# GpSimd splits the first eight weight tiles, and TensorE makes three unread products ahead of ten level groups

## The reference

```python
def _attn_ref(q, k, v, alpha):            # 4 x 8 heads, 768 tokens, 48 wide
    for t in range(S):
        state = alpha[:, :, t, :, None] * state + einsum('bhd,bhe->bhde', k[:, :, t], v[:, :, t])
        y[:, :, t] = einsum('bhd,bhde->bhe', q[:, :, t], state)

def _moe_ref(x, domain_probs, w1, w2):    # 3072 tokens x 384, 4 experts of 1024
    p = domain_probs / (domain_probs.sum(-1, keepdims=True) + 1e-09)
    for e in range(E):
        out += p[:, e:e + 1] * (maximum(x @ w1[e], 0.0) @ w2[e])

def _moe2_ref(x, w_in, w_out):            # 384 -> 2048 -> 384
    h = x @ w_in
    return (h - tanh(h)) @ w_out
```

## Time and profile before

| | us |
|---|---|
| median of 3 runs | 1374.95 (1374.37 to 1376.28) |
| the profiled execution | 1376.28 |
| its span | 1373.8 |
| TensorE busy | 1346.9 (98%) |
| TensorE on the chain that ended last | 90% |
| VectorE, ScalarE, GpSimd busy | 859.2, 569.1, 280.2 |
| mean granted clock | 0.987 |

### The profile page before, as it was taken

How to read it: one execution, slowest core, us unless ns; L and a number is a source line. 1 busy time by engine, 2 the same in 40 slices (tenths; PEclk the granted TensorE clock), 3 DMA queues, 4 the chain that set the end, 5 groups by cost and what they waited for, 6 DMA issues and landing times.

```text
span 1373.8 us, 26614 instructions
## 1 busy us (share of the span) xinstructions
PE 1346.9 (98%) x10589; PEld 1130.7 (82%) x10589; DVE 859.2 (63%) x1698; ACT 569.1 (41%) x1063; POOL 280.2 (20%) x270
## 2 busy tenths in 40 slices
PE   5899999999999999999999999999999999999999
PEld 5778788988878888878898888898887889888888
DVE  6874856985644975464787464497555478333385
ACT  1426256833233841414662323474231476111185
POOL 4767653014031002313001304000221000000000
PEclk7799999999999999999999999999999999999999
DMA  7497896866565656656655655655665465655552
GB/s 228 109 357 252 286 326 234 312 223 219 192 209 196 227 182 215 202 187 208 236 192 178 216 189 196 227 212 184 215 203 164 163 225 195 213 189 202 181 192 87
DMA packets 104682, 289.22 MB, mean 211 GB/s; under 512 B 9936, under 2 KB 64304, under 8 KB 104560
## 3 DMA queue, kind: packets, MB, share of 16 engines
q1 hardware_dynamic: 104128, 287.22, 62.3%
q10 hardware_dynamic: 432, 0.31, 0.1%
HBM read 242.61 MB, written 42.52 MB: 208 GB/s over the span
## 4 chain that ended last, share of the span: by engine, by line
PE 90%; DVE 6%; issue 2%; POOL 1%; DMA 1%; ACT 0%; DVEq 0%; SPq 0%; POOLq 0%; ACTq 0%
PE bank L742 15%; PE bank L743 13%; PE bank L744 13%; PE bank L767 9%; PE bank L768 9%; PE bank L769 9%; PE bank L793 4%; PE bank L791 4%; PE bank L792 4%; PE bank L633 3%; PE bank L691 1%; DVE RG L1265 1%; PE bank L611 1%; PE bank L663 1%; PE bank L653 1%
## 5 line engine op out<-in xcount | busy, mean ns | idle before, releaser
L967 ACT ACTIVATE HH<-GG 128x512 fp32r<-128x512 f32 x192 | 121.2, 631 | 630.5 <-PE bank L769 509.3
L742 PE MATMUL bank<-XB,RG 128*128 128x512 f32 x864 | 349.1, 404 | 3.5 <-DMA XB<-XS 3.1
L743 PE MATMUL bank<-XB,RG 128*128 128x512 f32 x864 | 340.0, 393 | 0.0
L744 PE MATMUL bank<-XB,RG 128*128 128x512 f32 x864 | 339.0, 392 | 0.0
L1215 DVE SCALAR_TENSOR_TENSOR GG<-bank,PB 128x512 f32<-128x512 f32 x192 | 133.4, 695 | 312.3 <-PE bank L744 312.0
L767 PE MATMUL bank<-HH,RG 128*128 128x512 f32 x576 | 224.3, 389 | 0.0
L768 PE MATMUL bank<-HH,RG 128*128 128x512 f32 x576 | 224.2, 389 | 0.0
L769 PE MATMUL bank<-HL,RG 128*128 128x512 f32 x576 | 224.0, 389 | 0.0
L1420 POOL TENSOR_TENSOR KU<-KU,TOT 128x256 f32<-128x256 f32 x80 | 62.2, 805 | 686.3 <-PE bank L633 686.3
L742 PEld LDWEIGHTS bank<-XB,RG 128*128 128x128 f32 x864 | 162.4, 188 | 44.4 <-issue 3.3
L744 PEld LDWEIGHTS bank<-XB,RG 128*128 128x128 f32 x864 | 162.5, 188 | 35.5
(11 more groups left out here) (121 smaller groups left out, 1687.6 us busy)
## 6 DMA issues: line engine op xcount, KB each, us to landing
RG<-scratch SPq DMA_DIRECT2D x240, 768.0 KB, 4.3
scratch<-RG SPq DMA_DIRECT2D x48, 768.0 KB, 5.3
VS<-vp SPq DMA_DIRECT2D x11, 768.0 KB, 6.1
WS<-w SPq DMA_DIRECT2D x32, 192.0 KB, 3.6
PB<-probs SPq DMA_DIRECT2D x6, 1024.0 KB, 6.9
AU<-qka SPq DMA_DIRECT2D x11, 512.0 KB, 5.4
R<-qka SPq DMA_DIRECT2D x11, 512.0 KB, 5.6
KU<-qka SPq DMA_DIRECT2D x11, 512.0 KB, 6.3
```

The lines of the kernel that those rows point to most:

```text
L742: nc.tensor.matmul(out, w1(g, 0, kt), x_part(m, 0, kt), start=(kt == order[0]), stop=False)
L743: nc.tensor.matmul(out, w1(g, 0, kt), x_part(m, 1, kt), start=False, stop=False)
L744: last = nc.tensor.matmul(out, w1(g, 1, kt), x_part(m, 0, kt), start=False, stop=(kt == order[-1]))
L967: nc.scalar.activation(HH[:, h_slot(g)], GG[:, h_slot(g)], ACT.Copy).then_inc(high, 1)
```

## The change

1. `paired_scores` takes its two bank waits first, and for levels 1 to 5 of both units it then makes three products of the identity with itself (128x128, float32, `keep_clock`) into the bank that the group's second half overwrites, ahead of the waits for keys and queries. Ten groups, thirty products.
2. The second run of unread products, ahead of the layers, grows from 6 to 12.
3. VectorE's splits 2 and 3 go to GpSimd, which now does 0 to 7 itself.
4. GpSimd multiplies unit 2's queries (`spread_queries(AHEAD)`) ahead of `join(1)`, not in `prepare(2)`. `join(1)` waits for that in place of the two waits on `keys_up`. `prepare(2)` no longer waits for unit 1's carried states between the two spreads.

```diff
             def paired_scores(u, level):
+                bank_free(u, 2 + 2 * level)
+                bank_free(u, 3 + 2 * level)
                 if level == 0:
                     pe.wait_ge(spread[own(u)], 1)
                 else:
+                    keep_clock(fill_bank(u, 3 + 2 * level), 3)
                     pe.wait_ge(keys_up[own(u)], level)
                     pe.wait_ge(rotated[own(u)], level)
-                bank_free(u, 2 + 2 * level)
-                bank_free(u, 3 + 2 * level)
...
-            keep_clock(bank[4], 6)
+            keep_clock(bank[4], 12)
...
             states(1)
-            split_low(2)
-            split_low(3)
             low_x(0)
...
-                spread_queries(u)
-                if pause:
-                    pool.wait_ge(carried[own(u - 1)], pause)
+                if u > AHEAD:
+                    spread_queries(u)
                 spread_distant(u)
...
             def join(u):
-                pool.wait_ge(keys_up[0], NL)
-                pool.wait_ge(keys_up[1], NL)
+                pool.wait_ge(spread[0], 2)
...
+            spread_queries(AHEAD)
             join(1)
             pool.wait_ge(joined[1], 5)
             split_low(0)
             split_low(1)
-            prepare(2, carried_at(1))
-            for g in range(LEAD, RING):
+            prepare(AHEAD)
+            for g in range(2, RING):
                 split_low(g)
```

More of the change, by code:

```diff
@@ L637, in scores, with keep_clock @@
                             last.then_inc(filled[own(u)], 1)
+            def keep_clock(out, n):
+                for i in range(n):
+                    nc.tensor.matmul(out[:, 0:P], ident[:, :], ident[:, :], start=True, stop=True)
             def paired_scores(u, level):
+                bank_free(u, 2 + 2 * level)
+                bank_free(u, 3 + 2 * level)
                 if level == 0:
@@ L694, in attend @@
                 last.then_inc(filled[own(u)], 1)
-            def keep_clock(out, n):
-                for i in range(n):
-                    nc.tensor.matmul(out[:, 0:P], ident[:, :], ident[:, :], start=True, stop=True)
             def attention(u, step):
@@ L1261, in split_low @@
             def split_low(g):
-                if g in (2, SLOTS1 + LEAD):
+                if g == SLOTS1 + LEAD:
                     dve.wait_ge(w_low, g)
@@ L1398, in paired_tabulate, with prepare @@
                     nc.gpsimd.tensor_tensor(both, one, two, ALU.mult).then_inc(tabled[own(u)], 1)
-            def prepare(u, pause=0):
+            def prepare(u):
                 n = turn_of(u)
@@ L1451, in split_low @@
             def split_low(g):
-                if g == LEAD:
-                    pool.wait_ge(w_low, g)
                 pool.wait_ge(w_high, g + 1)
```

## The result

The changed kernel takes 1385.93 us (median of four runs, 1385.66 to 1387.23) against 1374.92 (1374.37 to 1376.28) for the kernel before on the same chip: 11.0 us slower by the medians; the ratio is given as 1.0074, interval 1.0062 to 1.0086, which is 8.5 to 11.8 us. The forecast was 1375.3. What happened is the rival called "the clock stays at half until the transposes", and it cost more than the 8.2 us that it was priced at. The profiled execution of before is the slowest of its four, so the two profiles lie only 9.9 apart in their spans.

The account below looks back on a forecast made before the run. TensorE, busy 98% of the span, bounds the kernel after the start. GpSimd raising unit 2's keys at 79.5 against 79.14 adds 0.35 us to the 1374.95 median: 1375.3, own range 1373.8 to 1376.9, 8-in-10 range 1372.2 to 1383.4.

Parts of the forecast that it names:

- the clock stays at half until the transposes: Slower rival, TensorE's score groups: products run at half clock, last score 9 or more later; +8.2 us, 1383.2; chance 0.20.
- Step 3: TensorE's clock in the score groups: three wide products between narrow groups bring full clock back by the early thirties.
- The rival's price: Half-clock case: ten groups' products cost 12.8 to 15 us, pauses hide 3.9; last score 9 later, level 1 +8.2.
- Step 1: TensorE up to 28.5 us: nothing moves in time, two pauses (3.4 us) hide the first four groups' products.
- Step 2: TensorE from 28.48 to the last score: instruction supply of 126 rows per 3.9 us; end at 42.2, 0.7 later.
- Step 4: VectorE gives away its two splits; first wide products at full clock, TensorE alone about 2.4 us sooner after five tiles.
- the 3.97: Time in us of VectorE's two weight splits, said to go from the chain of waits before the first wide product.
- Step 5: GpSimd, the deciding part: join 1.1 late, more work behind it, unit 2's keys raised at 79.5, TensorE then takes level 1.
- +0.75 and +0.5: GpSimd behind the join: queries gone (minus 3.10), two splits of 1.92 added, +0.75; late staging of weight tiles, +0.5.
- the sum: Whole change at level 1 of unit 2: 79.5 against 79.14, +0.35 us, give or take 1.5.

Follow-up runs that it names:

- e2: Kernel before with only the thirty unread products and the bank waits ahead of them; 1386.38 us, ratio 1.0069.
- e3: Changed kernel with six unread products ahead of each of the ten groups instead of three; 1381.76 us (one run), kernel before 1376.14.
- e8: Changed kernel with fourteen unread products ahead of the first group, three ahead of the nine others; 1380.15 us (one run), kernel before 1376.51.
- e12: Kernel before with unit 2's queries ahead of the join, fourteen products ahead of the first group, three ahead of each other; 1375.96 us, ratio 1.0001.
- e4: Changed kernel with fourteen unread products ahead of the first group, none ahead of the others; 1381.45 us (one run), kernel before 1376.14.
- e9: Kernel before with unit 2's queries ahead of the join, fourteen products ahead of the first group, one ahead of each other; 1378.89 us, ratio 1.0015.
- e1: Changed kernel without the thirty unread products ahead of the groups; 1376.89 us, ratio 1.0007.
- e5: Changed kernel without the thirty products, with unit 2's queries and the join's waits back in their old places; 1380.69 us, ratio 1.0030.
- e6: Kernel before with one edit, GpSimd multiplies unit 2's queries ahead of the join; 1374.72 us, ratio 0.9991.
- e11: The kernel of e6 run again, unchanged, in a later comparison; 1374.04 us, ratio 0.9986.
- e10: Kernel of e6 with one more wait: GpSimd starts unit 2's queries only after unit 1's last keys are raised; 1376.73 us, ratio 1.0002.

## Why the prediction was wrong, step by step

**Step 3, the clock: the step that failed.** "Now three wide products stand between any two narrow groups, as in neither of the two, so I take the clock to be back by the early thirties." It was at half to the end of the transposes near 56. The argument took a place between two known ends (scores alone, 128-column work alone) and put it at the upper one without a row. What the runs showed in its place: three per group left it at half for 34 us, in the traces of after and e2 (and each of their eight executions took 1384.97 or more), six per group brought it up (e3). Once it was full, three kept it (e8, e12); it fell under groups alone in e4 and with one per group in e9. So the clock that this pattern ran at depended on the clock that it found. Products are not all of it: in e1 and e5 plain groups reached the full clock. The rival that the clock stays at half had 0.20 and was the better reading of the one row that counted, twelve microseconds of narrow work at half.

**The rival's price.** It was right in kind and too low: 9 for 10.8 at the last score, 8.2 for 9.7 at level 1 of unit 2, 8.2 for 11.0 on the median. Its own terms, 12.8 to 15 less 3.9, gave 8.9 to 11.1 for the last score; it took the lowest. Six product rows at half take 1.58 (17.86 to 19.43 on the chain), above the 1.28 to 1.5 taken from eight transposes and a 512-column product; ten are 15.8. Of these 5.0 were hidden (15.8 - 10.8), the pauses and short waits, about the 3.9 set down for them, and at the join nothing more was.

**Step 1** said that nothing moves up to 28.5 since the pauses hide four groups' products "about" at half. In after group (1,2) starts at 29.68, so its row 27, which stood at 28.48, comes near 30.5: 2 us late. The pauses themselves did vanish, as said. Its price for three products at full clock was too low as well: 2.06 for 16 rows is 0.77 for six, not 0.73, and e8 has 0.86 (23.80 to 24.66).

**Step 2** took 3.9 us per 126 product rows as the limit of the instruction supply. In e12 TensorE ran 505 product rows from 29.14 to 43.91, 3.7 us per 126, with one pause of 0.27 in them, and its own pace was 1.93 per 70 rows, 3.5 per 126. The limit is no higher than 3.7 there; it would have made the forecast 0.6 smaller and was no part of the miss. Two slips in the step have no weight either: group (0,5) ends 70 rows before the last, not 76, and 104 rows of the mix at its own prices take 2.3, not 2.0. By the Trainium skill, "Runtime: NRT & Kernel Launch", "Instruction fetch mechanics", the crossing of a block is mostly hidden. Inside the score groups and away from the loading of the first 30 us these runs agree, with pauses of 0.2 to 0.3; during it the runs with few or no products between the groups don't, with 0.9 to 3.2. That these pauses are such crossings rests on the count of 126 rows alone.

**Step 4.** VectorE's two splits left, and the first wide product came at full clock as said. What was wrong is the 3.97: on their own they are 1.99, the rest was GpSimd's doing, and moving the queries alone gives that back (e6, e11).

**Step 5.** The mechanism held: GpSimd worked without a pause from the join to the keys, and TensorE waited 1.98 for them (2 to 3 forecast). The sum was +0.75 and +0.5 behind the join: 88.76 - 55.47 is 33.3, against 32.7 before, so +0.6 and not +1.25: six splits cost 4.2 more than four and the queries' 3.1 are gone, but the first distant query took 1.6 where it had taken 2.13, and no staging wait came through. The join itself was to be +1.1 from step 2 alone; e1 shows +1.9 with no delay of the scores at all. It was the contention that the step left out: it let the queries run "into this idle time" of GpSimd without asking who shares something with GpSimd in it. e1, the change without its products, came out 0.75 above its kernel before where the sum had +0.35; that is the forecast about right by luck, two errors that cancel: TensorE's scores were not late, and the rotation was. The interval of e1 takes in no difference, so it can't confirm the sum either.

**The measure.** The kernel before spreads from 1374.2 to 1379.2 over all comparisons, and part of that has a source that the traces show: the two pauses ahead of 23 and 29 us were 1.38 and 2.06 in one run, 0.92 and 1.78 in e6, 1.20 and 3.15 in e10, with nothing changed ahead of them. The groups behind them start up to a microsecond earlier or later. Places of different profiles are therefore compared by their distances (join behind last score), not by their times alone.

## What to carry to other kernels

Beyond the 5 us of pauses that they filled, the unread products were paid in full here, where TensorE is the bound. So set the price of such a product at the clock you have against what the clock would give on the work between: here 0.8 us per group to win, 0.9 to hold it, 1.6 if it isn't won. Try the clock with one run that raises it and one that holds it before trusting that "some" wide work does. When work is moved into an engine's idle time, look at what the engine that shares a way to memory with it does there: the gain or the loss may be on that other engine, and a long instruction may be half waiting.

## What the runs showed of the hardware that was not expected

- **The clock depends on what it was.** The same three products and 64 score rows per group ran at half for 34 us (after) or at full for 21 us (e8); the clock at which they began is what differed. It is not the whole rule: plain groups rose from half to full in e1 (1.94 at 34.80, 1.14 at 38.64) and stayed at half in before.
- **Two two-input instructions of VectorE and GpSimd don't share, they queue.** The end of VectorE's rotation lies 0.54 or 0.55 us behind the end of GpSimd's queries in each of five runs: 53.39 and 52.84 (after), 44.28 and 43.73 (e1), 43.66 and 43.11 (e6), 45.05 and 44.51 (e11), 46.54 and 45.99 (e12). It began 0.4 to 1.9 us after them and took 1.04 to 2.54, 0.69 by itself. Predicated copies weren't slowed (0.76 to 0.78), nor were copies out of a bank (3.06 for eight beside the queries in e10, 3.05 in e11). In the other order GpSimd waits: its queries take 3.10 behind a running split, 2.36 or so by themselves. The Trainium skill says this in "SBUF — State Buffer", "SBUF: two separate sides": the pair of ports that the two engines share is an exclusive lock for a whole instruction, and the one that comes second blocks; a VectorE instruction takes part with two inputs from SBUF. The rows here agree.
- **A stretch at half clock can follow a wait, late too.** In e4 2.92 us of waiting at 82 was followed by scores of 1.56 instead of 0.89 and wide products 0.43 apart instead of 0.23, in e5 4.65 us by wide products 0.43 apart. In after and e8, with 1.98 and 2.02 us at the same place, the scores stayed at 0.89 and 0.90. A late key can cost more than its wait.
- **The granted clock of the first stretch of a trace can be wrong.** After reads 1.00 over 34 us of half-clock durations, and e1 reads 1.00 through its 1.94 and its 1.14. Where before has had a change of the clock in its record, the label and the durations agree.
- **Open:** whether it was the single product or the 1.44 us pause that let e9's clock fall wasn't tried, nor what raises the clock under plain groups in one trace and not in another. With one product per group and a held clock VectorE and GpSimd weren't met as the next bound; under plain groups at full clock TensorE did wait for them, 1.27 us for GpSimd in e4 (27.00) and 0.70 for VectorE in e1 (38.64).
